# Attention and two MLPs on one core: one value unit moved ahead of the quarter score unit, two loads and one weight copy moved

## The reference, cut to what matters

```python
scores = (q @ k^T) / sqrt(64)                  # per batch and head, 448 x 448
scores = cap * tanh(scores / cap)
attn   = exp(scores - max) / (sum + 1e-9)
x      = (attn @ v), heads side by side        # 896 tokens x 768
x      = relu(x @ w_in1)^2 @ w_out1            # 768 -> 2048 -> 768
out    = silu(x @ w_in2) @ w_out2
```

## Time and profile before

| | |
|---|---|
| median of 3 runs | 543.65 us (543.34 to 544.69) |
| the profiled execution's own time | 543.38 us |
| its span in the trace | 541.6 us |
| TensorE busy | 530.9 us (98%), granted clock 0.998 |
| VectorE, ScalarE, GpSimd busy | 361.9, 261.0, 80.0 us |
| chain that ended last | PE 81%, POOL 10%, DVE 3% |

### The profile page before, as it was taken

The page is one execution under the profiler, slowest core; times in us unless marked ns, Lnnn a source line. Parts: engine busy times, 40 slices in busy tenths (PEclk is TensorE's granted clock), DMA queues, the critical chain, the costliest instruction groups (busy, mean ns, idle before and its releaser), DMA issues.

```text
span 541.6 us, 7075 instructions
## 1 busy us (share of the span) xinstructions
PE 530.9 (98%) x2616; PEld 439.8 (81%) x2616; DVE 361.9 (67%) x623; ACT 261.0 (48%) x404; POOL 80.0 (15%) x54
## 2 busy tenths in 40 slices
PE   7999999999999999999999999999999999999996
PEld 5233334799999999999998999999999999999995
DVE  3298787687678634667789835556855345568985
ACT  5999995155443333444444344444433144454230
POOL 1899999100000000000000000000000000000000
PEclk9999999999999999999999999999999999999999
DMA  8789601051202202422022024211210241020546
GB/s 225 203 229 222 188 15 31 29 154 42 79 0 79 58 2 60 136 58 78 0 79 60 0 59 136 59 41 37 71 50 16 59 136 41 19 79 10 120 65 89
DMA packets 82117, 42.17 MB, mean 78 GB/s; under 512 B 26784, under 2 KB 79008, under 8 KB 82080
## 3 DMA queue, kind: packets, MB, share of 16 engines
q1 hardware_dynamic: 77952, 40.32, 28.9%
q10 hardware_dynamic: 4096, 1.38, 1.1%
q0 software_dynamic: 32, 0.00, 0.0%
HBM read 38.93 MB, written 2.75 MB: 77 GB/s over the span
## 4 chain that ended last, share of the span: by engine, by line
PE 81%; POOL 10%; DVE 3%; issue 2%; DMA 2%; ACT 0%; ACTq 0%; POOLq 0%; DVEq 0%
PE banks L531 26%; PE banks L532 26%; PE banks L533 26%; POOL asum L418 4%; POOL asum L415 3%; POOL asum L422 3%; PE banks L461 1%; DVE w_hl L931 1%; PE banks L454 1%; DMA qk_raw<-in_q_dram 1%; DVE y L1011 1%; DMA qk_raw<-in_k_dram 1%; PE banks L482 0%; PE banks L473 0%; ACT g_hi L733 0%
## 5 line engine op out<-in xcount | busy, mean ns | idle before, releaser
L531 PE MATMUL banks<-x_hi,w_hl 128*128 128x448 f32 x384 | 140.7, 366 | 0.0
L533 PE MATMUL banks<-x_hi,w_hl 128*128 128x448 f32 x384 | 140.5, 366 | 0.0
L532 PE MATMUL banks<-x_lo,w_hl 128*128 128x448 f32 x384 | 140.5, 366 | 0.0
L531 PE MATMUL banks<-g_hi,w_hl 128*128 128x448 f32 x336 | 123.4, 367 | 0.2 <-DVE w_hl L931 0.2
L533 PE MATMUL banks<-g_hi,w_hl 128*128 128x448 f32 x336 | 123.2, 367 | 0.0
L532 PE MATMUL banks<-g_lo,w_hl 128*128 128x448 f32 x336 | 123.2, 367 | 0.0
L531 PEld LDWEIGHTS banks<-x_hi,w_hl 128*128 128x128 f32 x384 | 72.1, 188 | 7.6 <-issue 1.4
L533 PEld LDWEIGHTS banks<-x_hi,w_hl 128*128 128x128 f32 x384 | 72.1, 188 | 6.2
L532 PEld LDWEIGHTS banks<-x_lo,w_hl 128*128 128x128 f32 x384 | 72.1, 188 | 6.2
L926 DVE TENSOR_TENSOR w_hl<-w_raw,w_hl 128x768 fp32r<-128x768 f32 x32 | 32.0, 1000 | 57.5 <-ACT w_hl L682 57.4
L714 ACT ACTIVATE work<-banks 128x448 f32<-128x448 f32 x64 | 31.3, 541 | 77.4 <-PE banks L533 68.4
(11 more groups left out here) (66 smaller groups left out, 525.7 us busy)
## 6 DMA issues: line engine op xcount, KB each, us to landing
w_raw<-in_moe_w_in_dram SPq DMA_DIRECT2D x32, 384.0 KB, 3.4
w_raw<-in_moe_w_out_dram SPq DMA_DIRECT2D x24, 512.0 KB, 5.2
qk_raw<-in_k_dram SPq DMA_DIRECT2D x44, 112.0 KB, 2.9
qk_raw<-in_q_dram SPq DMA_DIRECT2D x44, 112.0 KB, 3.3
v_t<-in_v_dram SPq DMA_DIRECT2D x24, 96.0 KB, 3.6
out_dram<-rows SPq DMA_DIRECT2D x40, 56.0 KB, 2.2
qk_raw<-in_k_dram ACTq DMA_DIRECT2D x4, 112.0 KB, 3.1
qk_raw<-in_q_dram ACTq DMA_DIRECT2D x4, 112.0 KB, 3.9
```

The costliest lines, as they stand in the source:

```text
L531: pe.matmul(dst, hi[:, kk, :], mov_hi, start=start, stop=False, skip_group_check=onto)
L532: pe.matmul(dst, hi[:, kk, :], mov_lo, start=False, stop=False, skip_group_check=onto)
L533: return pe.matmul(dst, lo[:, kk, :], mov_hi, start=False, stop=stop, skip_group_check=onto)
```

## The change

- On TensorE, `output_first` loses v(j,1). In the loop for j = 3 to 11 the order becomes s(j,0), s(j,1), s(j,2), then `output_first` of pair j-1 with v(j-1,0) alone, s(j,3), sums(j-2), v(j-1,1), v(j-1,2), rest. The first two pairs and pair 11's output keep their order.
- On ScalarE `tile_high(0, 0, 1)` moves from behind pair 9 to behind pair 11.
- On SP `load_v(1)` and `load_v_x` move from behind `load_qk(2)` to behind `load_qk(3)`, and change places.

```diff
@@ sync: loads
             for j in range(2, PAIRS):
                 sp.wait_ge(s_turned, 4 * (j - 1))
                 load_qk(j)
-                if j % 2 == 0:
+                if j % 2 == 0 and j > 2:
                     load_v(j // 2)
-                if j == 2:
+                if j == 3:
                     load_v_x()
+                    load_v(1)
@@ tensor: output_first
                 wait(pe, s_x, j.n - 1)
                 pe.wait_ge(s_exp, 2 * j.n + 1)
                 values(j, 0)
-                values(j, 1)
@@
             def output(j):
                 output_first(j)
+                values(j, 1)
                 output_rest(j)
@@
             for j in range(2):
                 scores(At(0, j + 1), 0)
                 output_first(At(0, j))
+                values(At(0, j), 1)
                 for u in range(1, CW):
                     scores(At(0, j + 1), u)
@@
             for j in range(3, PAIRS):
-                for u in range(C):
+                for u in range(CW):
                     scores(At(0, j), u)
+                output_first(At(0, j - 1))
+                scores(At(0, j), CW)
                 sums(At(0, j - 2))
-                output(At(0, j - 1))
+                values(At(0, j - 1), 1)
+                output_rest(At(0, j - 1))
@@ scalar
             for j in range(PAIRS - 1):
                 weights(At(0, j))
-                if j in (7, 9):
-                    tile_high(0, 0, (j - 7) // 2)
+                if j == 7:
+                    tile_high(0, 0, 0)
             weights(At(0, PAIRS - 1))
+            tile_high(0, 0, 1)
```

## The result

The changed kernel takes 545.63 us (median of 9 runs, 545.59 to 547.30); beside it the kernel before took 543.88 (9 runs, 543.34 to 544.69). The ratio is 1.0046, 95% interval 1.0037 to 1.0055: slower by 0.46%, 2.0 to 3.0 us by the interval. The two medians alone are 1.75 us apart (1.0032), just under that interval; both say slower. The profiled execution took 545.63 us, its span is 543.8 us (541.6 before), granted clock 0.999. The forecast was 545.6 us, and slower.

What follows compares the result with a forecast made beforehand. GpSimd bound the kernel up to sums(10), then TensorE, with 0.95 us of slack; 0.80 (TensorE late at sums(10)) + 1.22 (tile_low held) = 2.0 us slower, 545.6 median, range 543.4 to 546.8 (likeliest 545.2 to 546.2, chance 0.47).

Steps and rivals of the forecast that it cites:

- The bound: At sums(10), where GpSimd hands over to TensorE: 0.95 us of slack; TensorE faster gains nothing, slower by more costs.
- The saving that was none: Idle 0.65 before s(j,3) is the tile-shape switch, not tanh; moving v(j-1,0) saves nothing in seven of nine iterations.
- The wait on x: v(j-1,0) waits for x of pair j-3, 5.67 us behind sums; even iterations stall 0.49, sums(10) comes 0.80 late.
- ScalarE and GpSimd: Later exp1 holds GpSimd's line 418 in pairs 5, 7, 8, 9 by 0.58 in all; pair 10 ends at 88.80.
- tile_low: VectorE's tile_low(0,0,0) is held by GpSimd's addition of pair 11, so hidden_first loads at 91.84, not 90.62: 1.22 us.
- hidden_first could load 0.90 later: TensorE step from sums(10) at 89.72 to hidden_first's load at 90.62, if not held: 0.90 us.
- Loads and tile_high: Moved load_qk(3), v_x, v(1) and tile_high(0,0,1): zero net cost; v_x lands by 22.1, 0.7 us in hand.
- rival A: No change, centre 543.6, chance 0.26: x chain does not bind, TensorE gains 0.84 + 2 x 0.53, waits at sums(10).
- B: 544.4 us, chance 0.17: x chain binds, but tile_low gets in ahead of GpSimd's line 415 of pair 11; 0.80 left.

Runs made afterwards that it cites:

- e2: Kernel before with only the moved loads and the moved tile_high, TensorE's order as before: 543.36 us, ratio 0.9994.
- e5: Changed kernel with sums(j-2) ahead of v(j-1,0) and s(j,3): 543.42 us, ratio 0.9998.
- e1: Kernel before with only TensorE's new order; loads and tile_high(0,0,1) stay where they were: 546.52 us, ratio 1.0051.
- e4: Changed kernel with v(j-1,0) ahead of s(j,3) only in odd iterations, at its old place behind sums in even ones: 543.85 us, ratio 1.0014.
- e3: Changed kernel with VectorE's tile_low(0,0,0) ahead of take_sums(9) instead of behind it: 544.54 us, ratio 1.0025.
- e6: Changed kernel with GpSimd's addition of pair 11 (line 416) cut into two instructions, one for each head: 545.06 us, ratio 1.0028.
- e8: Kernel before with moved loads and tile_high, hidden_first(0,0) ahead of sums(10), and tile_low(0,0,1) inside finish(10): 542.28 us, ratio 0.9978.

## Why the prediction was right

**The bound, right.** Sums(10) had 0.95 us of slack and no more. e2 and e5 make TensorE earlier and change nothing (0.9994, 0.9998, idle time before sums(10) up to 1.58 and 1.38); e1 and the changed kernel make it later and pay.

**The saving that was none, right.** The idle time before the quarter unit was put down to tanh, and it was the change of tile shape: behind the move the value unit has the same 0.65, with "issue" as its cause, and s(j,3) has 0.23. This is the trap of such a change: a saving read off a releaser that had long been done.

**The wait on x, right in size.** 5.67 us were worked out for the chain; v(2,0), the first to wait, loads at 30.15, less the 0.35 by which this trace starts later (12.44 - 12.09) 29.80, forecast 29.81; two even iterations are 14.10 apart (37.00, 51.10) against 14.12 forecast, the stall is 1.11 - 0.65 = 0.46 against 0.49. v(9,0) loads at 79.31, which less the 0.35 is 78.96; forecast 79.02. Sums(10) at 90.02 is 89.67 on the same scale; forecast 89.72. e5 shows the cause, e4 agrees.

**ScalarE and GpSimd, right.** The idle time before line 419 above the usual 0.13 sums to 0.17 + 0.11 + 0.40 + 0.06 = 0.74 in pairs 5, 7, 8 and 9, forecast 0.58; GpSimd ends pair 10 at 89.12, that is 88.77, forecast 88.80. The 0.16 of idle time more came back in a pace slightly quicker than the 6.84, so this hit is in part luck.

**tile_low, right in kind, 0.3 too large.** It was issued 0.50 behind the addition of pair 11 (forecast 0.55) and held to its end; e3 and e6 show both halves of that. But the step "hidden_first could load 0.90 later" took its 0.90 from a sums that stood behind a wait. Unheld it is 1.23 (e3), so TensorE's own term is 1.1 and tile_low's 0.9. The two errors cancel, and not by luck: the load of hidden_first is set by the end of tile_low alone, so how the 2.0 is split does not move the sum, and the run-ins differ by 2.01.

**Loads and tile_high, right at zero** (e2), but rival A was partly wrong: it let TensorE gain 0.84 from the earlier q of pair 3 and 0.53 twice from tanh, and e2 shows that in the old order tanh(3,0) takes all of the first, and that only one 0.53 comes back. It would have moved rival A's slack, not its time. v_x landed in 2.3 to 3.8 us, where 1.9 to 3.0 had been taken over from before; the last was issued at 19.2, so it was there by 23.0 at most, and rest started at 23.15 with only the 0.70 of the shape change. By that bound the margin was 0.15 us, not 0.7.

**The number, closer than the working.** The forecast added 1.95 us to a median of 543.65 for the kernel before. Beside the changed kernel that median was 543.88, and the difference 1.75, so that 545.6 was met to 0.03 us is luck; the difference was met to 0.2. The range of 543.4 to 546.8 also took in "no change", and the case that came true had been given 0.47. What bears the forecast out is the loads and the x_lo rows above, more than the number.

**The rivals.** A (no change) is what e5 is, once the chain is cut: GpSimd binds again (1.38 before sums(10)). E4 has the same time, but there TensorE arrives with no slack left. B (TensorE late, tile_low not held) is e3: 544.54, forecast 544.4.

## What to carry to other kernels

Moving a piece of work forward moves its waits forward too: list every semaphore ahead of it, and for each the chain that raises it, before crediting the hole it is to fill. Where two engines run at the same pace (here 6.82 and 6.84 us a pair), freeing one gains nothing (e2), and delaying it costs once its slack is used up, here 0.95 us; look instead for the place where one hands over to the other, and put independent work there (e8). Two instructions that keep each other out, as tile_low and the additions do here, have a price that depends on which starts first: tile_low took 0.95 us when it was 0.01 ahead (e4) and 2.41 when it was 0.50 behind, so a small shift elsewhere can add most of an instruction's length.

## What the runs showed of the hardware

- VectorE's subtraction of two SBUF inputs (128x768, 0.95 us alone) took 2.41, 2.79 and 1.45 us (changed kernel, e1, e6) behind a running GpSimd addition of 2.09, 2.10 and 1.14 us, always ending 0.82 us after it. The GpSimd instruction that came next lost 0.14, 0.5 and 0.7 us in turn (2.23, 2.61 and 1.87 where 2.09, 2.09 and 1.14 are usual), and the addition that started 0.01 us behind tile_low in e4 lost 0.8 (2.92).
- Four fp32 matmul instructions of one shape count 0.43 in weight loads right behind a wait or a change of shape and 0.75 elsewhere, so that sums(10) and the switch behind it count 0.90 where sums was held (before) and 1.23 where it was not (e3). Costs read from loads depend on what stood before.
- The start of the program jitters by up to 0.6 us between executions of all these kernels (first addition at 12.09 to 12.68), a third of the effect studied. Distances within a trace do not have it.
